# A fused attention and two-MLP kernel: a reordered opening, a later start of the first tile's attention, and a jump in TensorE's code

## What is computed

```python
f = sigmoid(f_logit)                       # batch 4, heads 8, 768 tokens, head size 48
for t in range(S):                         # gated linear attention
    state = f[t][:, None] * state + outer(k[t], v[t])
    y[t] = q[t] @ state
x = y as 3072 rows of 384
xn = x / sqrt(mean(x * x) + 1e-6) * rms_g
x = (silu(xn @ w_gate) * (xn @ w_val)) @ w_out      # 384 -> 1536 -> 384
h = x @ w_in                                        # 384 -> 2048
out = where(h >= 1, h, where(h <= -1, 0, (h + 1)**2 / 4)) @ w_out2
```

## Time and profile before

| | |
|---|---|
| median of three runs | 933.28 us |
| the profiled execution's own time | 932.01 us |
| its span, first to last instruction | 930.3 us |
| TensorE matmul busy | 920.9 us (99%) |
| VectorE busy | 555.4 us (60%) |
| ScalarE busy | 329.9 us (35%) |
| GpSimd busy | 15.3 us (2%) |
| mean granted TensorE clock | 0.999 |

### The profile page before, as it was taken

The page is one execution under the profiler, slowest core; times in us unless marked ns, Lnnn a source line. Parts: engine busy times, 40 slices in busy tenths (PEclk is TensorE's granted clock), DMA queues, the critical chain, the costliest instruction groups (busy, mean ns, idle before and its releaser), DMA issues.

```text
span 930.3 us, 18650 instructions
## 1 busy us (share of the span) xinstructions
PE 920.9 (99%) x7498; PEld 784.0 (84%) x7498; DVE 555.4 (60%) x975; ACT 329.9 (35%) x563; POOL 15.3 (2%) x35
## 2 busy tenths in 40 slices
PE   7999999999999999999999999999999999999998
PEld 4999999998888888888888888888888888888886
DVE  8987658757656575575555555445445545454453
ACT  4653333332223232332233434243333433433333
POOL 1000000000000000000000000000000000000000
PEclk9999999999999999999999999999999999999999
DMA  7822533532422442233313100000000000000000
GB/s 248 306 70 71 161 91 101 177 97 86 145 74 66 138 127 71 82 123 101 102 51 97 40 1 0 1 34 0 28 6 0 34 0 0 34 0 0 35 1 34
DMA packets 52276, 65.89 MB, mean 71 GB/s; under 512 B 14576, under 2 KB 42992, under 8 KB 52208
## 3 DMA queue, kind: packets, MB, share of 16 engines
q1 hardware_dynamic: 52064, 64.75, 21.9%
q10 hardware_dynamic: 144, 0.13, 0.0%
HBM read 51.43 MB, written 13.43 MB: 70 GB/s over the span
## 4 chain that ended last, share of the span: by engine, by line
PE 98%; DVE 1%; issue 1%; DMA 0%; ACT 0%; DVEq 0%
PE gate_ps L629 16%; PE val_ps L629 16%; PE acc L707 14%; PE acc L651 11%; PE gate_ps L695 11%; PE val_ps L695 11%; PE acc L711 7%; PE acc L655 5%; PE pair_ps L469 2%; PE y_ps L492 2%; PE y_ps L531 2%; PE pair_ps L520 1%; PE acc L722 0%; DVE after L1062 0%; DMA raw<-qkf_dram 0%
## 5 line engine op out<-in xcount | busy, mean ns | idle before, releaser
L993 ACT ACTIVATE raw<-raw,columns 128x512 f32<-128x512 f32 x96 | 69.4, 723 | 155.1 <-DVE raw L1453 155.1
L707 PE MATMUL acc<-high 128*128 128x512 f32 x282 | 109.7, 389 | 0.0
L707 PE MATMUL acc<-high,low 128*128 128x512 f32 x282 | 109.7, 389 | 0.0
L651 PE MATMUL acc<-high 128*128 128x512 f32 (+2 forms) x252 | 90.0, 361 | 0.0
L651 PE MATMUL acc<-high,low 128*128 128x512 f32 (+2 forms) x252 | 89.3, 358 | 0.0
L1000 ACT ACTIVATE high<-qd 128x512 fp32r<-128x512 f32 x96 | 60.7, 632 | 73.3 <-DVE qd L1458 73.3
L711 PE MATMUL acc<-low,high 128*128 128x512 f32 x282 | 79.2, 389 | 0.0
L1453 DVE TENSOR_SCALAR raw<-val_ps 128x512 f32<-128x512 f32 x48 | 33.2, 691 | 76.5 <-PE val_ps L695 76.5
L1453 DVE TENSOR_SCALAR raw<-gate_ps 128x512 f32<-128x512 f32 x48 | 33.1, 689 | 61.9 <-PE gate_ps L695 61.6
L1390 DVE TENSOR_TENSOR low<-qd,high 128x512 fp32r<-128x512 f32 x96 | 65.8, 685 | 5.7 <-ACT high L1000 5.1
L629 PE MATMUL gate_ps<-high 128*128 128x512 f32 (+2 forms) x249 | 65.0, 369 | 0.1
(11 more groups left out here) (153 smaller groups left out, 1698.8 us busy)
## 6 DMA issues: line engine op xcount, KB each, us to landing
raw<-qkf_dram SPq DMA_DIRECT2D x22, 770.0 KB, 4.8
x_all<-wb_dram SPq DMA_DIRECT2D x12, 576.0 KB, 6.7
kd_turn_dram<-after SPq DMA_DIRECT2D x19, 256.0 KB, 2.9
kd<-kd_turn_dram SPq DMA_DIRECT2D x76, 64.0 KB, 2.5
v_sb<-v_dram SPq DMA_DIRECT2D x23, 192.0 KB, 2.7
v_early<-v_dram SPq DMA_DIRECT2D x23, 192.0 KB, 2.6
out_dram<-x_all SPq DMA_DIRECT2D x5, 768.0 KB, 3.8
x_turn_dram<-x_all SPq DMA_DIRECT2D x19, 192.0 KB, 1.9
```

The costliest lines, as they stand in the source:

```text
L651: pe.matmul(acc[:, m, 0:width(i)], wb_part(w, j, 2, m), h_hi[:, j % 2, 0:width(i)], start=(j == 0 and w is w_hi), stop=False)
L707: pe.matmul(acc[:, m, 0:N2], wc_part(w, j, 1, m), h2_hi[:, j % 2, :], start=(j == 0 and w is w_hi), stop=False)
L993: nc.scalar.activation(act2_buf[:, j % 2, :], act2_buf[:, j % 2, :], ACT.Square, bias=half_col[:, :], scale=0.5).then_inc(square_ready, 1)
```

## The change

TensorE's opening: the banks change (`val_ps` for the transposes, `acc` for the scores of chunks 0 and 1, `gate_ps` for the outputs of chunk 1, under the name `second_y`); one warm-up matmul goes; in chunks 0 and 1 the updates come ahead of the wait for the masked scores; chunk 0, whose carried state is zero, has no state matmuls, and `y_ps` is set to zero instead; `turn_x(0)` comes behind `attend(1)`; a code place is set ahead of all. VectorE, ScalarE and SyncE follow: other orders in the opening, the second weight load behind a wait. In the first tile `DELAY` moves the attention by three slots and `WINDOW` is 8 instead of 9; the scan and the `decay_k` of chunk 2 take part in that.

```diff
-WINDOW = 9
+DELAY, WINDOW = 3, 8
 LINE, JUMP = 256, 4
+OPENING = 162
-WARM_START, WARM_SCORES, WARM_LAST = 2, 1, 2
+WARM_START, WARM_LAST = 2, 2
...
-        turned_x = gate_ps
-        turned_parts = val_ps, acc[:, 1, :], acc[:, 2, :]
+        turned_parts = [acc[:, k, :] for k in range(KM)]
+        second_y = gate_ps[:, 0:DM + 1]
+        first_scores = acc[:, 1:3, 0:2 * UP].rearrange("s r (a t) -> s r a t", a=NP // 2)
+        second_squares = scores[:, :, :, :].rearrange("p r h t -> p (r h t)")[:, 0:DM + 1]
...
                 load_wb(0)
-                load_wb(1)
                 for part, x in enumerate(v_second):
                     sp.dma_start(x, v[1, :, 0, part * DM:(part + 1) * DM]).then_inc(v_second_loaded, 16)
-                sp.wait_ge(qd_ready, 1)
+                sp.wait_ge(scores_made, 2)
+                load_wb(1)
                 load_raw(2)
...
                 def attend_state(n, c):
                     pe.wait_ge(wide_ready, n + 1)
-                    if n > 0:
+                    if n > 1:
                         pe.wait_ge(xs_ready, n)
...
                 def attend(n, c, scores_next=False):
-                    pe.wait_ge(scores_ready, n + 1)
+                    early_chunk = isinstance(n, int) and n < FIRST
+                    if not early_chunk:
+                        pe.wait_ge(scores_ready, n + 1)
...
-                    attend_state(n, c)
+                    if not early_chunk:
+                        attend_state(n, c)
...
                     mm.then_inc(update_made, 1)
+                    if early_chunk:
+                        if n > 0:
+                            attend_state(n, c)
+                        pe.wait_ge(scores_ready, n + 1)
...
-                        o = slot - WINDOW * c
+                        o = slot - DELAY - WINDOW * c
...
                     pe.wait_ge(f_loaded, 16)
+                    pe.addr_align(LINE, OPENING, max_nops=JUMP)
                     keep_warm(WARM_START)
-                    turn_kd(0, acc[:, 1, :])
+                    turn_kd(0, val_ps)
                     score_alone(0, 0)
-                    keep_warm(WARM_SCORES)
                     attend(0, 0)
-                    turn_kd(1, acc[:, 1, :])
+                    turn_kd(1, val_ps)
                     score_alone(1, 1)
-                    turn_x(0, turned_x)
                     attend(1, 1)
+                    turn_x(0, val_ps)
                     keep_warm(WARM_LAST)
...
@@ ScalarE, second_tile @@
-                        if o == 0 and c == 1:
+                        if o == 0 and c == 0:
+                            sigmoid_f(n)
+                        elif o == 0 and c == 1:
...
@@ ScalarE, the opening @@
                 split_wb(0)
-                round_x(0, 0, turned_x)
-                sigmoid_f(2)
                 square_sum(1)
+                round_x(0, 0, val_ps)
                 split_wb(1)
                 round_parts()
...
@@ VectorE, second_tile @@
-                        if o == 1 and c == 0:
-                            decay_k(n, c)
-                        elif o == 1:
+                        if o == (1 if c > 0 else 2):
                             decay_after(n, inputs)
-                        elif o == 3 and c > 0:
+                        elif o == (3 if c > 0 else 4):
                             decay_k(n, c, inputs)
...
                 nc.vector.memset(half_col[:, :], 0.5)
+                nc.vector.memset(y_ps[:, 0:DM], 0.0)
                 nc.vector.memset(y_ps[:, DM:DM + 1], (EPS * DM) ** 0.5)
+                nc.vector.memset(second_y[:, DM:DM + 1], (EPS * DM) ** 0.5)
...
                 decay_upto(1, 1, raw_second)
+                decay_q(1, 1, raw_second)
                 update_state(0)
-                decay_q(1, 1, raw_second)
                 decay_state(1, 1)
+                mask_scores(1)
                 dve.wait_ge(g_loaded, 16)
                 normalise(0)
-                mask_scores(1)
                 split_wb(0)
-                rest_x(0, 0, turned_x)
                 update_state(1)
-                decay_after(2)
+                rest_x(0, 0, val_ps)
                 normalise_parts()
```

More of the change, by code:

```diff
@@ L455, in score @@
                 def score(n, c):
+                    made = first_scores if isinstance(n, int) and n < FIRST else score_ps
                     for a in range(NP // 2):
@@ L463, in score @@
                                     rows = slice(r * HP, (r + 1) * HP)
-                                    to = score_ps[keys, r, a, :].rearrange("s (j t) -> s j t", t=HP)
+                                    to = made[keys, r, a, :].rearrange("s (j t) -> s j t", t=HP)
                                     if h == odd:
@@ L482, in score_alone, with outputs @@
                     score(n, c)
+                def outputs(n):
+                    return second_y[:, 0:DM].rearrange("t (r p e) -> t r p e", r=2, p=NP) if n == 1 else y_heads
                 def attend_state(n, c):
                     pe.wait_ge(wide_ready, n + 1)
-                    if n > 0:
+                    if n > 1:
                         pe.wait_ge(xs_ready, n)
@@ L491, in attend_state @@
                             q = slice(s * QW, (s + 1) * QW)
-                            pe.matmul(y_heads[q, :, p, :], qd[0:PR, half(n, c), p, q],
+                            pe.matmul(outputs(n)[q, :, p, :], qd[0:PR, half(n, c), p, q],
                                       wide[0:PR, p, :].rearrange("d (r e) -> d r e", r=2),
@@ L527, in attend @@
                                 if odd is None:
-                                    y, t, given = y_heads[q, r, 2 * a:2 * a + 2, :], s * QW, early[:, r, a, :]
+                                    y, t, given = outputs(n)[q, r, 2 * a:2 * a + 2, :], s * QW, early[:, r, a, :]
                                 else:
-                                    y, t, given = y_heads[q, r, 2 * a + odd, :], s * QW + odd * HP, values[:, r, 2 * a + odd, :]
+                                    y, t, given = outputs(n)[q, r, 2 * a + odd, :], s * QW + odd * HP, values[:, r, 2 * a + odd, :]
                                 mm = pe.matmul(y, scores[:, r, a, t:t + QW], given,
@@ L790, in square_sum @@
                     act.wait_ge(y_made, n + 1)
+                    if isinstance(n, int) and n == 1:
+                        act.wait_ge(xs_ready, 1)
+                        nc.scalar.activation(second_squares, second_y, ACT.Square, scale=DM ** -0.5, accum_out=ssq[:, :])\
+                            .then_inc(ssq_ready, 1)
+                        return
                     if isinstance(n, int) and n < CARRIED:
@@ L1028, in _ @@
                 sigmoid_f(1, raw_second)
-                copy_kdT(0, acc[:, 1, :])
+                copy_kdT(0, val_ps)
                 square_sum(0)
-                copy_kdT(1, acc[:, 1, :])
+                copy_kdT(1, val_ps)
                 widen(1)
                 split_wb(0)
-                round_x(0, 0, turned_x)
-                sigmoid_f(2)
                 square_sum(1)
+                round_x(0, 0, val_ps)
                 split_wb(1)
@@ L1130, in mask_scores @@
                         dve.wait_ge(y_made, n)
-                    nc.vector.tensor_tensor(scores[:, :, :, :], score_ps,
+                    nc.vector.tensor_tensor(scores[:, :, :, :], first_scores if isinstance(n, int) and n < FIRST else score_ps,
                                             causal[:, :].unsqueeze(1).unsqueeze(1)
@@ L1149, in normalise_parts @@
                     dve.wait_ge(rstd_ready, 2)
+                    dve.wait_ge(xT_made, 1)
                     for k in range(KM):
                         columns = slice(k * P, (k + 1) * P)
-                        nc.vector.scalar_tensor_tensor(out=xs[:, columns], in0=y_ps[:, columns], scalar=rstd[:, :],
+                        nc.vector.scalar_tensor_tensor(out=xs[:, columns], in0=second_y[:, columns], scalar=rstd[:, :],
                                                        in1=g_rows[:, columns], op0=ALU.mult, op1=ALU.mult)\
```

## The result

The changed kernel took **935.11 us** in the median of 11 runs (934.35 to 937.8), the kernel before 932.44 beside it: the ratio is 1.0032, interval 1.0024 to 1.004. It is slower, by 2.7 us. The same kernel in a second set took 935.83 in the median of 6 runs, 3.5 over the kernel before (experiment 8), so the medians of this kernel are good to some 0.7 us. The profiled execution took 936.01 us with a span of 934.3, against 932.01 of the kernel before. One run of one experiment, the 1313.3 us of `e_gap_warm`, ran at a mean granted clock of 0.655 and is left out of its ratio.

The account below looks back on a forecast made before the run. TensorE bounds the kernel after the first tile; in that tile VectorE is full beside it. Scores of chunk 4 come 2.98 later, less 1.08 for one group: 1.90 on the median 933.28 gives 935.2, range 932.5 to 937.0.

Parts of the forecast that it names:

- The opening's 1.8 us: Opening, before the first gate: chunk 1 done at 16.6 instead of 18.45, 1.8 us sooner, including the 0.51 pause.
- The weight load takes it away: Opening: load_wb(1), now behind scores_made 2, lands at 18.8 after 4.1; of 1.8 us 0.58 is left, gate at 20.37.
- VectorE's sum in the first tile: First tile: 1.14 scan, 2.06 other work and 0.67 idle added ahead of decay_q(4), at 59.68 instead of 56.39.
- TensorE's wait for `decay_q(4)`: First tile: TensorE's longest wait, 1.5 us, ahead of the scores of chunk 4, which start near 60.5.
- The early sign: First tile: rest_h(1) comes behind two scans, so TensorE waits some 0.4 ahead of the scores of chunk 2.
- 1.90 later at the end of the tile: First tile's end: scores of chunk 4 start 2.98 later, less 1.08 for one matmul group fewer behind them.
- Nothing differs beyond 75 us: Behind the first tile, past 75 us: the two traces were expected to run side by side.
- The slots are harmless: Rival, first tile: VectorE's queue has enough give and TensorE never waits; 932.7, or up to 931.5; chance 0.20.
- The weights are late: Rival, opening: weights land in 6.7 instead of 4.1, everything from the rounding on 2.6 later; 937.8; chance 0.09.
- The clock: Rival, opening and first tile: the granted clock falls, 1 us may show on the tile; 936.2; chance 0.04.
- Another pause: Rival, first tile: a pause of 0.5 to 0.8 behind the line with chunk 2's attention; 935.2 to 936; chance 0.05.

Follow-up runs that it names:

- e_gap_warm: e_gap with one more group of throwaway warm-up matmuls on TensorE ahead of chunk 1's scores: 931.93 us, ratio 0.9994.
- e_scan_sooner: e_gap_warm with step 1's weights loaded ahead of chunk 2's raw data and chunk 2's scan sooner on VectorE, ahead of tile 0's rest_x: 931.79 us, ratio 0.9995.
- e_wb_early: The changed kernel with the second weight load issued ahead of chunk 1's values again, not behind the wait for the scores: 934.49 us, ratio 1.0026.
- e_before_slots_new: The kernel before with only the change's slots, DELAY, WINDOW = 3, 8: 934.55 us, ratio 1.0026.
- e_q_early: The changed kernel with only chunk 4's query product and decayed state moved back from slot 26 to 25: 936.12 us, ratio 1.0047.
- e_split_behind: The changed kernel with VectorE's weight split of step 8 moved behind slot 26: 933.78 us, ratio 1.0013.
- e_after_warm: The changed kernel with one more group of throwaway warm-up matmuls ahead of chunk 1's scores: 935.63 us, ratio 1.004.
- e_slots_old: The changed kernel with the slots of before, DELAY, WINDOW = 0, 9: 933.68 us, ratio 1.0019.
- e_no_jump: The changed kernel without the code place (the jump) in front of TensorE's opening: 935.63 us, ratio 1.0035.
- r_after: The changed kernel once more, unchanged, in a second set: 935.83 us, ratio 1.0034.
- e_gap: The changed kernel's opening with the loads and slots of before, and chunk 2's scan in the opening behind normalise_parts: 933.16 us, ratio 1.0006.
- e_three: The changed kernel with the edits of e_split_behind, e_wb_early and e_gap_warm at once: 933.27 us, ratio 1.0011.

## Why the prediction was right, and where it wasn't

The number, 935.2 against 935.11 (935.83 in the second set), and the sign are right. By its steps:

- **The opening's 1.8 us.** Right. Product of chunk 1 at 12.87, scores at 13.70, both as worked out; the next group at 16.58, where I had 16.6. The pause of 0.51 is gone from the path. The changed kernel shows none under the mask either; that one there costs nothing, `e_scan_sooner` bears out, with a pause of 0.41 that delays nothing.
- **The weight load takes it away.** The mechanism is right, shown by `e_wb_early`; the size is off. Landing took 4.5 instead of the 4.1 that I took from the short end of the earlier trace rows, so the gate gained 0.27 and not 0.58. What `e_wb_early` adds: with the weights in time the gate still starts only 0.9 sooner than before, at 20.05, with the turned values (L613) as the next thing that ScalarE waits for.
- **VectorE's sum in the first tile.** The busy part is right: 34.55 + 1.14 + 2.06 = 37.75 forecast, 37.99 measured. The idle part was too small: 0.27 + 0.67 forecast, 1.52 measured. From 21.18 that gives 60.69 for the product where I had 59.68. The wait that I had counted, ahead of the mask of chunk 3, is there, 0.68. What the sum lacked stands mostly at the head of the tile, 0.30 for a value product and 0.18 for the third weight block, as in `e_before_slots_new`, where it was 0.88: attention moved to later slots leaves VectorE idle where it had stood.

```profile
48.41 0.96 DVE L1151 TENSOR_TENSOR scores<-pair_ps,causal 128x768 f32<-128x768 f32 x1 [0.68 <-PE pair_ps L473]
```

- **TensorE's wait for `decay_q(4)`.** A wait of 1.14 where I gave 1.5, and its cause was told by half. `e_q_early` shows that moving the product alone gains nothing, because `rest_x(3)` is as late; `e_split_behind` shows that moving the split, which is ahead of both, removes the wait and gives 1.3. The early sign, 0.4 ahead of the scores of chunk 2, came as 0.21.
- **1.90 later at the end of the tile.** The step that was mis-sized: 2.91 in the profile. The 1.01 between is just what VectorE's product for chunk 4 lacks: 0.19 by its start (21.18, not 20.99), 0.24 by its work, 0.58 by its idle time. The medians of the runs, 2.7 and 3.5 over the kernel before, lie on both sides of the 2.9. The forecast of the time still fits because I set it on 933.28, the median then known: before measured 932.44 in the same set as the change, 0.84 lower. A shift 0.8 too small on a base 0.8 too high is luck, and the ratio forecast, 935.2/933.28 = 1.0021, lies below the measured 1.0024 to 1.004.
- **Nothing differs beyond 75 us.** Wrong, in both profiled executions of the changed kernel: 1.1 us were lost at 183 to 191 us, and `e_after_warm` shows the same long wait (7.10). No other trace has a wait over 5.1 there. The forecast had nothing for this, and by what mechanism the change brings it stays open.

The rivals. *The slots are harmless* has fallen: alone they cost 2.3 us (`e_before_slots_new`). *The weights are late*: the second block to 4.5, not 6.7. The third block is another matter: where ScalarE waited for it, 0.75 us in `e_slots_old`, 1.38 in `e_no_jump` and 1.95 in `e_after_warm`, TensorE waited in turn, and the forecast did not look at it. *The clock*: it does fall in some executions, in the opening (`r_after`, 0.2 us at the gate) and in the first tile where TensorE has waited for long (`e_slots_old`). For the changed kernel itself no gain of the warm-up group is seen (`e_after_warm`), but the clock is what put `e_gap` above the kernel before. *Another pause* came just where it was counted, at 40.84 in the line with the attention of chunk 2, with 0.49 us, and it seems absorbed as I said: the wait for the queries of chunk 3 that `e_no_jump` shows isn't there. I gave it 0.05; it came in every profiled kernel with the jump and the new slots, with 0.28 to 1.04. The rule cited in the prediction from the Trainium skill ("Runtime: NRT & Kernel Launch", Instruction fetch mechanics) is that such crossings are mostly hidden. The changed kernel's trace agrees: 550 matmuls and 550 weight loads stand ahead of the pause at 40.84, which from place 162 and with the waits is by my estimate the fifth crossing, and the first four show no pause.

Do the prices overlap? By the marks they do: the slots alone cost 2.31 (`e_before_slots_new`), the rest without the slots 3.03 in an execution of which the clock took perhaps 1.3 to 1.8 (`e_slots_old`), together 2.91 and not 3.5 or more. By the medians, 2.3 and 1.5, they do with the 2.7 of the first set and hardly with the 3.5 of the second, in which the third tile's 1.1 may be contained. Both make TensorE wait for the same engine; that the waits cover each other is what I read from it, not what a run shows by itself.

Open: why the store of the turned values takes 4.5 us instead of 1.9 at 173 us in these executions (4.1 in `e_split_behind` and `e_three`), why the third weight block lands late in some, and what the jump is worth, 0 to 1 us.

## What to carry to other kernels

Where two engines both work 99% of a stretch, write down the order of the queue of the one that isn't the bound, and count what the edit puts ahead of each result that the other waits for. Count every result of that slot, not only the one whose name is in the wait: here two came late together, and only moving what stood ahead of both helped. And a chain made shorter gives nothing if its end hangs on a load whose issue was tied to it; look where the load is asked for before the gain is counted.

## What the runs showed of the hardware

- The granted clock fell from 1.00 to 0.50, from 2.4 to 1.2 GHz, for 3.4 us in some executions of a kernel and not in others. In both traces that caught it TensorE had been idle for 1.4 to 1.6 us between small products (12.25 to 13.69 in `r_after`, 25.85 to 27.42 in `e_slots_old`); in the first the fall came at the end of the gap, in the second some 1.7 us behind it. In the changed kernel's first profile the same gap of 1.45 left the clock at 1.00. A fall went with some 1.3 to 1.8 us in the full first tile and cost 0.2 under the wait for the weights. Two matmuls of 128x512 put in the gap removed it in ten runs, and with it 1.2 us of the median.
- The start of an execution differs too. The 32 matmuls of the scores of chunk 0 took 0.95 us in most profiles and 1.20, 1.36, 1.47 and 1.61 in `e_split_behind`, `e_wb_early`, `e_after_warm` and `e_gap_warm`, though the view grants 1.00 there. In `r_after` the 32 of chunk 1 took the same 1.61 at a granted clock of 0.50. The opening is up to 0.7 us late by it, so a late instruction in one profile need not come from the edit.
- A pause of TensorE's sequencer at one place of its code differed in length: 0.49 and 0.48 in the two profiles of the changed kernel, 0.28 in `e_wb_early`, 1.04 in `e_split_behind`, and 0.66 in `e_three`, where it fell six matmuls earlier. All stand in the line (256 instructions, `LINE`) with the attention of chunk 2. I had taken one size, 0.5.
- The same store of 192 KB, whose 19 issues land in 1.9 us in the middle, took 4.4 to 4.5 us once in the third tile, in three executions (the row of the changed kernel; the kernel before had 3.6 at most, the other profiles 3.7 to 4.1):

```profile
DMA to landing us min/median/max: 1.8/1.9/4.5
```
